# FFN2 in a channel-attention + FFN kernel: seven block products per pair in place of eight, with the factors of w_out streamed from DRAM

## The reference, cut to what matters

```python
# q, k, v: (2, 6016, 256) f32; w_in (256, 2048), w_out (2048, 256)
s = kn.transpose(0, 2, 1) @ qn / tau      # channel attention: 256 x 256 scores per batch
a = softmax(s); x = (v @ a).reshape(12032, 256)
h = x @ w_in
g = h * (1.0 / (1.0 + np.exp(-h)))        # SiLU
return (g @ w_out).astype(np.float32)
```

## Time and profile before

| | us |
|---|---|
| median of 3 runs | 1074.14 (1074.05 to 1074.95) |
| span of the profiled execution | 1072.1 |
| TensorE matmul busy | 1067.7 |
| DVE busy | 730.0 |
| ACT busy | 633.9 |
| POOL busy | 62.0 |

### The profile page before, as it was taken

One profiled execution on the slowest core, in us unless ns is written; L12 is line 12 of the kernel. 1 busy time (PEld: TensorE's weight loads), 2 busy tenths in 40 slices (PEclk: granted clock), 3 DMA queues, 4 the chain that ended last, 5 costly groups with the idle time before them and its releaser, 6 DMA issues.

```text
span 1072.1 us, 13055 instructions
## 1 busy us (share of the span) xinstructions
PE 1067.7 (100%) x4848; PEld 902.5 (84%) x4848; DVE 730.0 (68%) x941; ACT 633.9 (59%) x789; POOL 62.0 (6%) x33
## 2 busy tenths in 40 slices
PE   9999999999999999999999999999999999999998
PEld 8988888888888888888999888888888888888998
DVE  6889787567566566566788776667567566566665
ACT  7998665555555555555666655555555555555554
POOL 3792000000000000000000000000000000000000
PEclk9999999999999999999999999999999999999999
DMA  9991000200200200200200200200200200200100
GB/s 358 397 362 40 1 1 1 79 1 1 79 1 0 78 0 0 73 0 0 79 1 1 74 1 1 79 1 1 79 1 1 78 0 0 73 0 0 40 1 35
DMA packets 26365, 54.08 MB, mean 50 GB/s; under 512 B 2512, under 2 KB 6864, under 8 KB 26320
## 3 DMA queue, kind: packets, MB, share of 16 engines
q1 hardware_dynamic: 25888, 52.86, 13.5%
q10 hardware_dynamic: 432, 0.62, 0.2%
HBM read 41.16 MB, written 12.32 MB: 50 GB/s over the span
## 4 chain that ended last, share of the span: by engine, by line
PE 99%; DMA 0%; SPq 0%; ACT 0%; issue 0%
PE ps_o L530 16%; PE ps_o L531 16%; PE ps_o L529 16%; PE ps_h L496 14%; PE ps_h L495 14%; PE ps_h L494 14%; PE ps_o L434 5%; PE ps_o L449 1%; PE ps_o L456 1%; DMA qk<-k_dram 0%; PE ps_h L486 0%; PE ps_h L488 0%; PE ps_h L487 0%; PE ps_o L487 0%; PE ps_o L486 0%; PE ps_o L488 0%
## 5 line engine op out<-in xcount | busy, mean ns | idle before, releaser
L496 PE MATMUL ps_h<-b_hi,a_lo_rest 128*128 128x512 f32 (+1 forms) x504 | 194.1, 385 | 0.0
L495 PE MATMUL ps_h<-b_lo,a_hi_rest 128*128 128x512 f32 (+1 forms) x504 | 194.1, 385 | 0.0
L494 PE MATMUL ps_h<-b_hi,a_hi_rest 128*128 128x512 f32 (+1 forms) x504 | 194.0, 385 | 0.0
L978 DVE TENSOR_TENSOR h_b<-ps_h,u 128x512 f32<-128x512 f32 x96 | 66.4, 692 | 162.2 <-PE ps_h L496 162.1
L956 DVE TENSOR_TENSOR u<-ps_h,u 128x512 f32<-128x512 f32 x96 | 66.4, 692 | 142.4 <-PE ps_h L496 91.2
L750 ACT ACTIVATE h_a<-ps_h 128x512 f32<-128x512 f32 x96 | 57.4, 598 | 162.6 <-PE ps_h L496 162.6
L530 PE MATMUL ps_o<-g_lo_a,wo_hi 128*128 128x512 f32 (+1 forms) x384 | 147.9, 385 | 0.0
L529 PE MATMUL ps_o<-g_hi_b,wo_hi 128*128 128x512 f32 (+1 forms) x384 | 147.9, 385 | 0.0
L531 PE MATMUL ps_o<-g_hi_b,wo_lo 128*128 128x512 f32 (+1 forms) x384 | 147.9, 385 | 0.0
L529 PE MATMUL ps_o<-g_hi_a,wo_hi 128*128 128x512 f32 (+1 forms) x384 | 147.9, 385 | 0.0
L530 PE MATMUL ps_o<-g_lo_b,wo_hi 128*128 128x512 f32 (+1 forms) x384 | 147.8, 385 | 0.0
(11 more groups left out here) (138 smaller groups left out, 1602.1 us busy)
## 6 DMA issues: line engine op xcount, KB each, us to landing
v_raw<-v_t_dram SPq DMA_DIRECT2D x40, 256.0 KB, 3.7
out_t_dram<-v_raw SPq DMA_DIRECT2D x20, 512.0 KB, 3.2
qk<-q_dram SPq DMA_DIRECT2D x17, 384.0 KB, 10.8
qk<-k_dram SPq DMA_DIRECT2D x17, 384.0 KB, 11.8
wp_raw<-q_dram SPq DMA_DIRECT2D x7, 384.0 KB, 10.4
wp_raw<-k_dram SPq DMA_DIRECT2D x7, 384.0 KB, 11.8
w_in_raw<-w_in_dram SPq DMA_DIRECT2D x4, 512.0 KB, 11.8
wo_raw<-w_out_dram SPq DMA_DIRECT2D x4, 512.0 KB, 12.3
```

Source lines behind the costliest of these rows:

```text
L494: nc.tensor.matmul(ps_h[:, bank, 0:n], w_hi, x_hi, start=start, stop=False, skip_group_check=True)
L495: nc.tensor.matmul(ps_h[:, bank, 0:n], w_hi, x_lo, start=False, stop=False, skip_group_check=True)
L496: return nc.tensor.matmul(ps_h[:, bank, 0:n], w_lo, x_hi, start=False, stop=stop, skip_group_check=True)
```

## The change

The first step stays at eight output products, in a new order. From the second step on the second product is done with seven, too. Its right factors are g's four blocks, of which two are taken with the opposite sign, and their sums (T1, T3, T2, T4 of g); its left factors F1 to F7 are blocks of w_out and their sums. They do not fit in SBUF, so POOL makes them once (`part`), SP stores them in a DRAM tensor (s_dram), and for each pair SP loads the pair's seven factors, high and low, into one of two ring slots (`load_ring_a`, `load_ring_b`). Six of the seven results are added up over the pairs of a step in six PSUM banks. The seventh (f21) has none of its own: it goes into bank Y of the first product, and each pair DVE adds it to fl in SBUF (`add_flush`; for a step's first pair ACT copies it). At the end of a step the six sums are copied out by ACT and combined, in part by DVE (`sum_u`, `make_nv`, `sum_c22`) and in part by accumulating DMAs from POOL into the output in DRAM. The first product now uses two banks, X and Y: U1 is copied from X to Y by ACT (`seed_u1`), and P6, P5, P3 and P2, P4 are added on top by TensorE. The sums of v's blocks are made by accumulating DMAs from POOL. The second batch's raw factors are saved to DRAM, loaded back pair by pair (`load_a1`) and summed and rounded by POOL (`prepare_a1`). The loops over steps are written out.

The new code's core; SWITCH is 40, FIRST 8, the index n counts pairs from 0 to 95:

```diff
+            def second(n, factor, x_hi, x_lo, out, start, tok):
+                w_hi, w_lo = ring[:, n % 2, 0, factor, :], ring[:, n % 2, 1, factor, :]
+                nc.tensor.matmul(out[:, 0:tok], w_hi, x_hi[:, 0:tok], start=start, stop=False, skip_group_check=True)
+                nc.tensor.matmul(out[:, 0:tok], w_hi, x_lo[:, 0:tok], start=False, stop=False, skip_group_check=True)
+                return nc.tensor.matmul(out[:, 0:tok], w_lo, x_hi[:, 0:tok], start=False, stop=True,
+                                        skip_group_check=True)
...
+            def pair_step(n):                                  # TensorE
+                wait_for_step(n)
+                p1(n, pair, par, tok)
+                if n > FIRST + 1:
+                    f_t1(n - 2)
+                f22(n - 1)
+                p6(n, pair, par, tok)
+                p2(n, pair, par, tok)
+                f11(n - 1)
+                p5(n, pair, par, tok)
+                p7(n, pair, par, tok)
+                if n > FIRST + 1:
+                    f_t2(n - 2)
+                p3(n, pair, par, tok)
+                p4(n, pair, par, tok)
+                f_t4(n - 1)
+                f_t3(n - 1)
+                pe.wait_ge(c21_made, n + 1)
+                f21(n - 1)
...
+            ROUND_X = {2: (B11, B21), 3: (B22,), 4: (T2,), 5: (T1,), 6: (T3,), 7: (T4,)}
+            def pair_step(n):                                  # ACT
+                if n - 2 >= FIRST and pair == 2:
+                    flush(n - 2)
+                round_h(n - 1, before, H21, silu_21)
+                seed_u1(n, tok)
+                round_t13(n - 1, before)
+                if it > 1 and pair == 1:
+                    copy_m7(it - 1)
+                copy_u(n, tok)
+                round_t4(n - 1, before)
+                silu_c11(n, tok)
+                round_h(n, tok, H11, silu_11)
+                copy_w(n, tok)
+                if it > 1 and pair == 0:
+                    copy_m3(it - 1)
+                    copy_m1(it - 1)
+                if it > 1 and pair == 1:
+                    copy_m4(it - 1)
+                    copy_m5(it - 1)
+                if it < FINAL:
+                    for block_ in ROUND_X.get(pair, ()):
+                        round_x(it + 1, block_, block_)
+                round_t2(n - 1, before)
+                silu_c22(n, tok)
+                silu_c12(n, tok)
+                round_h(n, tok, H22, silu_22)
+                silu_c21(n, tok)
...
+            SPLIT_X = {3: (B11,), 4: (B21,), 5: (B22, T2), 6: (T1, T3), 7: (T4,)}
+            PARTS_AT = {2: (0, 1), 3: (2,), 4: (3,), 6: (4,), 8: (5,), 10: (6,), 12: (7,)}
+            def first_step(n):                                 # DVE, n < 8
+                if n:
+                    split_h(n - 1, TOK, H11)
+                    split_h(n - 1, TOK, H21)
+                if 1 <= n < PAIRS - 1:
+                    split_a(0, n + 1)
+                if n in SPLIT_X_FIRST:
+                    split_x(1, *SPLIT_X_FIRST[n])
+                make_c22(n, TOK)
+                split_h(n, TOK, H22)
+                for i in PARTS_AT.get(n, ()):
+                    split_part(i)
+                make_c21(n, TOK)
+                split_h(n, TOK, H12)
+                if n < PAIRS - 2:
+                    sum_a(0, n + 2)
...
+            def pair_step(n):                                  # DVE
+                if n - 2 > FIRST and (n - 2) % PAIRS:
+                    add_flush(n - 2)
+                sum_t2(n - 1, before)
+                split_h(n - 1, before, H21)
+                if it > 1 and pair == 2:
+                    sum_u(it - 1)
+                if it > 1 and pair == 3:
+                    make_nv(it - 1)
+                if it > 1 and pair == 4:
+                    sum_c22(it - 1)
+                sum_t4(n - 1, before)
+                split_t13(n - 1, before)
+                split_t4(n - 1, before)
+                if it < FINAL:
+                    for block_ in SPLIT_X.get(pair, ()):
+                        split_x(it + 1, block_, block_)
+                split_h(n, tok, H11)
+                make_c22(n, tok)
+                split_t2(n - 1, before)
+                make_c21(n, tok)
+                for i in PARTS_AT.get(n, ()):
+                    split_part(i)
+                if n - 1 in reload_at:
+                    split_a1(reload_at[n - 1])
+                sum_t13(n, tok)
+                split_h(n, tok, H22)
...
+            for n in range(FIRST + 2, PERIODS):                # SP
+                load_ring_a(n)                                 # waits for f21(n - 2)
+                if it > 1 and pair == 0:
+                    begin_c12(it - 1)
+                if it > 1 and pair == 1:
+                    begin_c21(it - 1)                          # waits for o4_copied
+                if it > 1 and pair == 4:
+                    store_c22(it - 1)
+                if pair == PAIRS - 1 and it + 2 < ALL:
+                    sp.wait_ge(x_split, 3 + FACTORS * it)
+                    load_x(it + 2)
+                load_ring_b(n)                                 # waits for f_t2(n - 2)
+                if n + 1 in reload_at:
+                    load_a1(reload_at[n + 1])                  # waits for a1_split of the pair before
...
+            for n in range(FIRST + 2, PERIODS):                # POOL
+                if it > 1 and pair == 1:
+                    store_flushed(it - 1)
+                    add_o7(it - 1)                             # waits for c21_begun
+                    add_o1(it - 1)                             # sum_u waits for o1_stored
+                if it > 1 and pair == 2:
+                    add_u(it - 1)
+                if it > 1 and pair == 3:
+                    add_nv(it - 1)
+                if pair == 2 and it + 1 < ALL:
+                    add_x_first(it + 1)
+                if pair == 3 and it + 1 < ALL:
+                    add_x_second(it + 1)
+                if pair == 6 and it + 1 < ALL:
+                    add_x_third(it + 1)
+                if n in reload_at:
+                    prepare_a1(reload_at[n])
```

More of the change, by code:

```diff
@@ L331, in _ @@
[L331 to L339 removed]
+            load_x(1)
@@ L583, in _, with closing_products @@
+            def closing_products(n):
+                f_t1(n - 1)
+                f22(n)
+                f_t2(n - 1)
+                f11(n)
+                f_t1(n)
+                f_t2(n)
+                f_t3(n)
+                pe.wait_ge(fl_added, flushed_by(n - 1))
+                f21(n)
+                f_t4(n)
             pe.wait_ge(consts_made, 1)
@@ new lines, in turning_pair @@
+            def turning_pair(n):
+                silu_c21(n - 1, TOK)
+                round_h(n - 1, TOK, H21, silu_21)
+                seed_u1(n, TOK)
+                copy_out(1, 0)
+                copy_u(n, TOK)
+                silu_c11(n, TOK)
+                copy_w(n, TOK)
+                copy_out(1, 1)
+                silu_c22(n, TOK)
+                silu_c12(n, TOK)
+                round_h(n, TOK, H22, silu_22)
+                copy_out(0, 0)
+                silu_c21(n, TOK)
+                round_h(n, TOK, H11, silu_11)
```

1197 lines of the change are left out of this document (838 added, 359 removed).

## The result

The changed kernel takes 1197.47 us (median of 4 runs, 1196.7 to 1198.93), against 1074.18 of the kernel before in the same comparison: ratio 1.1148, 95% interval 1.1132 to 1.1164, or 123 us slower. The direction was right and the size was not: the forecast was 1115 and the range ended at 1152.

A forecast was written before the change was run, and what follows sets the result against it. The prediction took TensorE's string of matmuls as the bound: 1074.1 - 58.7 for removed matmuls, + 27 + 15 + 6 + 12 + 26 + 12 + 2 for added work and waits = 1115 us; range 1066 to 1152.

The forecast's parts named there:

- removed matmuls: From step two the second product takes 21 matmuls a pair for 24; 88 pairs change, saving 58.7 us.
- (a): In pairs 6 and 7 p4 waits for make_c22, behind DVE's split_x waiting for ACT's round_x: 27 us.
- (b): DVE's loop takes 9.55 us a pair against PE's 9.53; extra operations in pairs 3 to 5 cost 15 us.
- (c): ACT's copies out of PSUM in pairs 0 and 1 and pair 2's second round_x delay round_t2: 6 us.
- (d): In pair 2 DVE's sum_u waits for o1's accumulating transfer, sent behind o7 and taken as 4.0 us: 12 us.
- (e): Second batch's factors: DVE's splits, POOL's sums blocking DVE, one hold-up of SP: 26 us, from 5 to 41.
- (f): Making w_out's factors on POOL and DVE, mainly PE waiting for H12's split in step one: 12 us, 5 to 22.
- (g): The turn at pair 8 and the last chain, t4's sum, round and split ahead of f_t4: 2 us.
- (h): Sums of v's blocks moved to POOL's accumulating transfers, and load_x's six transfers for four, stay hidden: nothing.
- rival 3: The accumulating transfers are late, 8 us in place of 4, 40 us in all: 1155 us; chance 14%.
- rival 1: Faster: DVE's loop closes under 9.53 us a pair and PE stays the bound: 1058 us; chance 16%.
- rival 2: POOL and DVE don't hold each other up in short operations, 15 less in (e), 5 in (f): 1095 us; 17%.

The follow-up runs named there:

- experiment 1: POOL sends o1 ahead of o7 instead of behind it, against the changed kernel: 1132.44 us, ratio 1.0539 to the kernel before.
- experiment 4: Second batch's own factors left out (loads, sums, splits, waits), against the changed kernel: 1175.26 us, ratio 1.0956 to the kernel before.
- experiment 6: On experiment 1's kernel, SP issues all eight loads of the second batch's factors one pair later: 1130.16 us, ratio 1.0519 to the kernel before.
- experiment 5: On experiment 1's kernel, ACT rounds T1 and T3 one pair earlier and T4's split stands behind split_t2: 1113.01 us, ratio 1.0372 to the kernel before.
- experiment 12: On o1 ahead of o7, roundings earlier and one factor load later: roundings and splits of x spread over other pairs from step 2; 1108.71 us.
- experiment 11: On o1 ahead of o7, roundings earlier and one factor load later: POOL's sums for the second batch's factors left out; 1099.21 us.

## Why the prediction was wrong

The forecast was 1115 and the time 1197: slower, as I said, and 82 us further, outside my range. Its steps beside what the runs and pair lengths show (us, on the time of the whole kernel):

| step | priced | measured | from |
|---|---|---|---|
| removed matmuls | -58.7 | -58.7 | 4584 left, spacing 0.2265 |
| (a) round_x in pairs 6, 7 | 27 | 31 | 1.53 above 9.53, twice, 10 steps |
| (b), (c) DVE's loop, ACT's copies | 21 | 23 | pairs 0 to 5 above 9.53 |
| **(d) sum_u waits for o1** | **12** | **65** | experiment 1 |
| (e) second batch's factors | 26 | 22 | experiment 4 |
| (f) w_out's factors and new order of step 0 | 12 | 18 | steps 0 and 1 |
| (g) turn and last chain | 2 | 9 | before the first copy 1.9, behind the last 7.2 |
| (h) load of x | 0 | 7 | pair 2 of step 1 |

They add up to 116 of the 123; 7 are not attributed.

**(d) is the step that failed**, by 53 of the 82 us that I was off. Its start was right within half a microsecond: o4 is copied 6.5 us into pair 1, its store seen landed 2.6 later (2.1 forecast), the two issues 0.57 apart (0.7 forecast). What failed is "nearest is a 256 KB transfer with an idle queue, 3.7; with 4.0". One accumulating transfer does take 4.0; but I had just written that o1 goes "only behind add_o7", and priced o1 as if it were alone. It took 7.8 (median), which put `sum_u` at 7.9 of the pair (from 398.96), where rival 3 with its 8 us had 7.7. So rival 3 was right on the transfer, given 14%; its reason, that they queue behind each other, is a part at best (step 5 of the kernel after, experiments 1 and 6). And the range that I gave ended at 1152, short of this rival's own 1155. The rival too came out short, 52 us for this term where experiment 1 shows 65: it charged only the wait, and what stands behind, TensorE's clock at the lower level for some eight to twelve matmuls, is another 1.6 to 2.6 us each time. Also P7 stood still through ACT's `round_t4`, a queue that my list of what waits behind `sum_u` ("t4's sum, three splits and c22") did not follow onto ACT. The Trainium skill (DMA: Bandwidth & Descriptors, Anatomy of one DMA) gave an estimate of 2.6 us here; with nothing ahead in its queue the transfer takes 4.0 (kernel after) to 5.0 (experiment 1), both medians, and the measurement decides.

**(a) held**, mechanism and size: p4 waits longest in pairs 6 and 7 (1.17 and 1.18 in step 3), DVE for round_x ahead of it, and experiment 5 took back 19 of the 31. What it could not take back is the splits' own work.

**(b) and (c) held** to a tenth: 10.03, 10.03 and 10.23 in pairs 3 to 5 where 9.53 plus 0.5, 0.5 and 0.6 was forecast. That kills rival 1: pairs 3 to 5 ran at 10.0 to 10.2, and the shortest with one operation added to DVE's 14, pair 6 of experiment 12, at 9.62. DVE over 85% busy came out as 80% for the span, 83% in step 3, and 90% once the stalls had gone (73.7 of 81.8 us in step 3 of experiment 1).

**(e) held**: 22 for 26, 11 of it POOL's sums. Rival 2, that POOL and DVE don't hold each other up, is refuted by experiment 11. The rule of the Trainium skill (SBUF, Who interferes with whom), that two SBUF inputs on DVE and a GpSimd operation exclude each other, agrees in kind; its full price, 41, does not: DVE lost 8.6 us of busy time and the kernel 11, not the whole of POOL's time.

**(f) was too small, its mechanism right.** In the kernel after TensorE waits at `output` for the split of H12 behind every pair of step 0 that has a split_part in it (pairs 2, 3, 4 and 6), and behind no other; the last line is step 1:

```profile
139.62 0.69 DVE L1511 TENSOR_TENSOR parts<-parts 128x512 fp32r<-128x512 f32 x1 [2.53 <-POOL parts L621]
...
142.03 0.79 PE L844 MATMUL ps_o<-g_hi,wo_hi 128*128 128x512 f32 x1 [5.03 <-DVE g_lo L1543]
...
167.35 0.50 PE L844 MATMUL ps_o<-g_hi,wo_hi 128*128 128x512 f32 x1 [0.80 <-DVE g_lo L1543]
...
170.14 0.53 ACT L1080 ACTIVATE a_hi_last<-wp_raw 128x384 fp32r<-128x384 f32 x1 [1.63 <-DMA s_dram<-parts]
...
171.72 0.50 PE L799 MATMUL ps_h<-b_hi,a_hi_mid 128*128 128x512 f32 x1 [0.64 <-ACT u L1144]
...
189.89 0.50 PE L844 MATMUL ps_o<-g_hi,wo_hi 128*128 128x512 f32 x1 [0.80 <-DVE g_lo L1543]
...
231.09 1.15 ACT L1126 ACTIVATE b_hi<-x_raw 128x512 fp32r<-128x512 f32 x2 [5.63 <-DMA x_raw<-v_t_dram]
```

A single part costs 0.80 to 0.81, less than the 1.08 that I had put. The two parts of pair 2 cost 5.03: DVE waited 2.53 for POOL's rounding of the second, which I had not seen as a wait at all, and the lower clock followed (nine spacings of 0.43). Pair 5 has no part and is 1.2 us longer than before: ACT's `round_a` waits 1.63 for the store of a part, the copy of u is queued behind it, and TensorE waits 0.64 for that (171.72). That store was in no term of mine. The 1.4 and 1.3 us that the first two pairs of step 0 are longer are not followed.

**(h), "nothing", held in nine steps and failed in one.** The last line above is step 1: SP issued step 2's x only behind the store of a part of w_out, the load of the next and the stores of step 0's outputs, and ACT waited 5.63 us. I had looked at the issue in pair 7 and not at the one-off in step 1.

**(g)**: the last matmul begins 9.3 us before the end of the span where it was 3.5 before; the last sums, seven DVE operations in a row, stand there uncovered.
